# First group's diagonal sums from products by channel on TensorE, and SyncE's loads of later groups in another order

## The reference, cut to what matters

```python
# attention, per batch and head, token by token
kt, vt, rt, wt = k[t], v[t], r[t], w[t]
y[t]  = rt @ (state + outer(u * kt, vt))
state = wt[:, None] * state + outer(kt, vt)
# first block
h = x @ w_in
x = knee(h) @ w_out        # 0 below -1, h above 1, (h + 1)^2 / 4 between
# second block
out = (silu(x @ w_gate) * (x @ w_val)) @ w_out2
```

## Time and profile before

| | us |
|---|---|
| median of 3 runs | 955.78 |
| lowest and highest run | 955.15, 956.08 |
| the profiled execution | 956.56 |
| its span | 954.8 |
| TensorE busy | 934.9 |
| VectorE busy | 553.4 |
| ScalarE busy | 392.3 |
| GpSimd busy | 166.4 |

### The profile page before, as it was taken

One profiled execution on the slowest core, in us unless ns is written; L12 is line 12 of the kernel. 1 busy time (PEld: TensorE's weight loads), 2 busy tenths in 40 slices (PEclk: granted clock), 3 DMA queues, 4 the chain that ended last, 5 costly groups with the idle time before them and its releaser, 6 DMA issues.

```text
span 954.8 us, 20721 instructions
## 1 busy us (share of the span) xinstructions
PE 934.9 (98%) x8344; PEld 918.9 (96%) x8344; DVE 553.4 (58%) x975; ACT 392.3 (41%) x827; POOL 166.4 (17%) x155
## 2 busy tenths in 40 slices
PE   6899999999999999999999999999999999999997
PEld 5889999999999999999999999999999999999997
DVE  8998877777778778764444433333343343434333
ACT  5675545455454555535674322222222222222222
POOL 5993220402104022020444100000000000000000
PEclk9999999999999999999999999999999999999999
DMA  9825453443523435322334010010101001010000
GB/s 306 247 85 181 117 155 117 119 150 116 187 85 116 143 102 161 116 58 88 103 86 119 21 50 1 1 50 1 50 0 49 0 0 49 0 49 0 25 1 27
DMA packets 49715, 79.58 MB, mean 83 GB/s; under 512 B 14784, under 2 KB 35648, under 8 KB 49632
## 3 DMA queue, kind: packets, MB, share of 16 engines
q1 hardware_dynamic: 49632, 78.42, 26.1%
HBM read 60.71 MB, written 17.69 MB: 82 GB/s over the span
## 4 chain that ended last, share of the span: by engine, by line
PE 91%; DVE 5%; issue 2%; ACT 0%; DMA 0%; POOL 0%; DVEq 0%; POOLq 0%
PE bank L1437 50%; PE bank L1465 35%; PE bank L1496 2%; PE bank L1527 2%; PE bank L1522 1%; DVE suf L1130 1%; PE bank L1514 1%; DVE k_r_by_channel L1155 0%; DVE k_r_by_channel L1152 0%; DVE gate L1279 0%; DVE glo L1272 0%; DVE att L1197 0%; DVE diag L1160 0%; DMA w_by_channel<-in_w_channel 0%; DVE att L1203 0%
## 5 line engine op out<-in xcount | busy, mean ns | idle before, releaser
L969 ACT ACTIVATE ghi<-gate 128x384 fp32r<-128x384 f32 x224 | 117.3, 524 | 209.7 <-DVE gate L1291 95.4
L1272 DVE TENSOR_TENSOR glo<-gate,ghi 128x384 fp32r<-128x384 f32 x224 | 136.8, 611 | 83.0 <-ACT ghi L969 81.2
L1289 DVE TENSOR_TENSOR gate<-bank,gate 128x384 f32<-128x384 f32 x96 | 53.5, 558 | 215.0 <-ACT gate L1090 215.0
L1437 PE MATMUL bank<-xhi,w2gv_ahi 128*128 128x384 f32 x480 | 161.3, 336 | 0.0
L1437 PE MATMUL bank<-xlo,w2gv_ahi 128*128 128x384 f32 x480 | 161.3, 336 | 0.0
L1437 PE MATMUL bank<-xhi,w2gv_alo 128*128 128x384 f32 x480 | 161.3, 336 | 0.0
L1090 ACT ACTIVATE gate<-bank 128x384 f32<-128x384 f32 x96 | 47.2, 492 | 227.7 <-PE bank L1437 227.7
L1465 PE MATMUL bank<-ghi,w1ohi 128*128 128x384 f32 x384 | 132.8, 346 | 1.0 <-DVE glo L1272 1.0
L1437 PE MATMUL bank<-xhi,w1ihi 128*128 128x384 f32 x384 | 129.6, 337 | 1.4 <-issue 0.9
L1437 PE MATMUL bank<-xhi,w1ilo 128*128 128x384 f32 x384 | 129.4, 337 | 0.0
L1465 PE MATMUL bank<-glo,w1ohi 128*128 128x384 f32 x384 | 129.4, 337 | 0.0
(11 more groups left out here) (105 smaller groups left out, 1506.6 us busy)
## 6 DMA issues: line engine op xcount, KB each, us to landing
r_k_v_by_token<-in_rkv_token SPq DMA_DIRECT2D x21, 672.0 KB, 5.2
k_r_by_channel<-in_kr_channel SPq DMA_DIRECT2D x18, 512.0 KB, 3.9
w_by_channel<-in_w_channel SPq DMA_DIRECT2D x24, 226.2 KB, 3.6
k_blocks_out<-k_blocks SPq DMA_DIRECT2D x18, 256.0 KB, 2.6
k_moved<-k_blocks_out SPq DMA_DIRECT2D x72, 64.0 KB, 2.0
x_t<-ring SPq DMA_DIRECT2D x8, 576.0 KB, 3.2
x_raw<-x_t SPq DMA_DIRECT2D x8, 576.0 KB, 4.0
ring<-in_w_out SPq DMA_DIRECT2D x21, 192.0 KB, 2.9
```

The costliest lines, as they stand in the source:

```text
L969: e.activation(ghi[j % 2][:, :], gate[j % 2][:, :], ACT.Copy).then_inc(M["hi", ph], 1)
L1272: e.tensor_tensor(glo[j % 2][:, :], gate[j % 2][:, :], ghi[j % 2][:, :].bitcast(F32), ALU.subtract)\
L1289: e.tensor_tensor(q, hid[j % 2][:, 0:T], q, ALU.mult).then_inc(M["t", 2], 1)
L1437: m = e.matmul(out, w_of(a, k), x_of(b_, k), start=start and i == 0, stop=stop and i == total - 1)
```

## The change

For the first group alone the sums are made another way. VectorE multiplies r with k by channel, before either is scaled (`r_times_k`). The product lies in the place of r and k by token, which are no longer loaded for this group. After the four transposes of a KT fill, TensorE makes four more matmuls into the same bank: the product as stationary side, and as moving side two columns of a new input `u_of_head` (112 x 4 x 2 numbers), so that 2 sums per pair of heads come out. ScalarE copies them to `diag` behind its copy of k. GpSimd's two products and VectorE's reduction fall away for this group; chunk 3 goes back to GpSimd.

```diff
+        def r_k_of(w):
+            return tok[0:PR, w, 2 * DM - NPAIR * WIN:2 * DM].rearrange("q (p t) -> q p t", p=NPAIR)
...
-                used = 3 * DM if first(g) else 3 * DM + DM // 2
-                e.dma_start(tok[:, w, 0:used], tok_d[g, w][:, 0:used]).then_inc(ld["tok", w], 16)
+                used = slice(2 * DM, 3 * DM) if first(g) else slice(0, 3 * DM + DM // 2)
+                e.dma_start(tok[:, w, used], tok_d[g, w][:, used]).then_inc(ld["tok", w], 16)
...
             load_kr(0, 1)
+            e.dma_start(pick[:, :, :], pick_d).then_inc(ld["pick"], 16)
             load_tok(0, 0)
-            e.dma_start(uu[:, :], u_d).then_inc(ld["u"], 16)
             load_w(0, 2)
             load_kr(0, 2)
             load_tok(0, 1)
-            load_w1(1)
+            load_w1(2)
             load_tok(0, 2)
-            load_w1(RING - 1)
+            load_w1(RING - 2)
+            e.dma_start(uu[:, :], u_d).then_inc(ld["u"], 16)
...
                 then_load(load_w, 1)
+                then_load(load_kr, 0)
+                then_load(load_tok, 0)
                 move_x(g, 0)
-                then_load(load_kr, 0)
                 move_k(g, 2)
-                then_load(load_tok, 0)
                 then_load(load_w, 2)
+                move_x(g, 1)
+                move_x(g, 2)
                 for w in (1, 2):
-                    move_x(g, w)
                     then_load(load_kr, w)
                     then_load(load_tok, w)
...
-            diag_products(0, 0)
-            diag_products(0, 1)
             diag_values(0, 0)
-            diag_products(0, 2)
+            w1_lo(0)
+            diag_values(0, 1)
+            w1_lo(1)
             decay_second()
-            diag_values(0, 1)
             diag_values(0, 2)
...
                     e.activation(ktk[:, :], src[:, 0:NPAIR * PR], ACT.Copy).then_inc(kt_out, 1)
+                    if first(g):
+                        e.activation(dg[:, w, :], src[:, NPAIR * PR:NPAIR * PR + H], ACT.Copy).then_inc(diag_d, 1)
...
+            more_hi(2)
             drain(0, fill_no(0, "KT", 2), 0)
...
+            def r_times_k(w):
+                e.wait_ge(ld["kr", w], 16)
+                e.tensor_tensor(r_k_of(w), kr[:, w, 1, :, :], kr[:, w, 0, :, :], ALU.mult).then_inc(r_k, 1)
...
             for w in range(2):
                 scan_window(0, w)
+                r_times_k(w)
                 scale_window(0, w)
-            diag_sum(0, 0)
             drain_at(0)
             scan_window(0, 2)
+            r_times_k(2)
             scale_window(0, 2)
...
-            diag_sum(0, 1)
-            diag_sum(0, 2)
             drain_at(2)
...
-            w1_lo(DVE_CHUNK)
             suffix_scan(1, 0)
...
                         m = e.transpose(out[:, p * PR:(p + 1) * PR], kr[:, w, 0, p, :], ident[0:PR, 0:PR])
+                    if first(g):
+                        e.wait_ge(r_k, w + 1)
+                        e.wait_ge(ld["pick"], 16)
+                        for p in range(NPAIR):
+                            c0 = NPAIR * PR + 2 * p
+                            m = e.matmul(out[:, c0:c0 + 2], r_k_of(w)[:, p, :], pick[:, p, :], start=True, stop=True)
```

More of the change, by code:

```diff
@@ L114 @@
 SCAN_SLOTS_FIRST = {11: 0, 13: 1, 14: 2}
-DVE_CHUNK = 3
 HI_FIRST = {0: 13, 1: 13, 2: 15, 3: 18, 4: 21, 5: 24, 6: 27, 7: 30, 8: 32}
@@ L152, in fill_no, with build_program @@
     return fills(g).index((kind, w, n))
-def build_program(nc, w_d, kr_d, tok_d, u_d, cst_d, w1i_d, w1o_d, w2g_d, w2v_d,
+def build_program(nc, w_d, kr_d, tok_d, u_d, pick_d, cst_d, w1i_d, w1o_d, w2g_d, w2v_d,
                   w2o_d, rs_d, ks_d, vs_d, ws_d, us_d, out_d, x2_d, ys_d, kb_d, xb_d):
@@ L233, in build_program @@
         dg, _ = place("diag", [P, NW, H], F32)
+        pick, _ = place("u_of_head", [PR, NPAIR, 2], F32)
         assert at[0] <= flag_at
@@ L271, in sem @@
             return ctx.enter_context(nc.semaphore(name))
-        ld = {n: sem(f"ld_{n}") for n in ("cst", "u")}
+        ld = {n: sem(f"ld_{n}") for n in ("cst", "u", "pick")}
         ld.update({(n, w): sem(f"ld_{n}{w}") for n in ("w", "kr", "tok") for w in range(NW)})
@@ L276, in build_program @@
         raw2 = [sem(f"raw2_{i}") for i in range(RING2)]
-        whi, wlo, wlo_d = sem("whi"), sem("wlo"), sem("wlo_d")
+        whi, wlo = sem("whi"), sem("wlo")
         whi2, wlo2 = sem("whi2"), sem("wlo2")
@@ L284, in build_program @@
         diag_d = sem("diag_d")
+        r_k = sem("r_k")
         fill = sem("fill")
@@ L331, in wait_lo @@
         def wait_lo(wait, c):
-            if c == DVE_CHUNK:
-                wait(wlo_d, 1)
-            else:
-                wait(wlo, c + 1 if c < DVE_CHUNK else c)
+            wait(wlo, c + 1)
         def bank_of(g, f):
@@ L836, in w1_lo @@
             def w1_lo(c):
-                if c == DVE_CHUNK:
-                    return
                 t = w1i if c % 2 == 0 else w1o
@@ L842, in diag_products @@
             def diag_products(g, w):
-                n = (g * NW + w) * OPS_DIAG
+                n = ((g - 1) * NW + w) * OPS_DIAG
                 rk = r_tok(w)
@@ L864, in decay_second @@
                 e.wait_ge(st_out, 2 * w)
-                e.wait_ge(diag_p, NW * OPS_DIAG)
                 for i in range(2):
@@ L872, in decay_second @@
                 e.wait_ge(st_dec, OPS_DECAY * (w + 1))
-            diag_products(0, 0)
-            diag_products(0, 1)
             diag_values(0, 0)
-            diag_products(0, 2)
+            w1_lo(0)
+            diag_values(0, 1)
+            w1_lo(1)
             decay_second()
-            diag_values(0, 1)
             diag_values(0, 2)
             for c in range(2 * J1):
-                w1_lo(c)
+                if c > 1:
+                    w1_lo(c)
                 if c in PRODUCTS_AT:
@@ L1158, in diag_sum @@
             def diag_sum(g, w):
-                e.wait_ge(diag_p, (g * NW + w) * OPS_DIAG + 2)
+                e.wait_ge(diag_p, ((g - 1) * NW + w) * OPS_DIAG + 2)
                 e.tensor_reduce(dg[:, w, :], r_tok(w).rearrange("p (h d) -> p h d", d=D), AX.X, ALU.add)\
@@ L1244, in turn_k @@
                 if n == 0:
-                    e.wait_ge(wlo, 2 * J1 - 1)
-                    e.wait_ge(wlo_d, 1)
+                    e.wait_ge(wlo, 2 * J1)
                 else:
@@ L1304, in _ @@
             e.wait_ge(zero_p, 3)
-            def w1_lo(c):
-                t = w1i if c % 2 == 0 else w1o
-                e.wait_ge(whi, c + 1)
-                e.wait_ge(raw[c % RING], 16 * (c // RING + 1))
-                e.tensor_tensor(t[1][:, c // 2, :], chunk_raw(c), t[0][:, c // 2, :].bitcast(F32),
-                                ALU.subtract).then_inc(wlo_d, 1)
+            def r_times_k(w):
+                e.wait_ge(ld["kr", w], 16)
+                e.tensor_tensor(r_k_of(w), kr[:, w, 1, :, :], kr[:, w, 0, :, :], ALU.mult).then_inc(r_k, 1)
             def drain_at(w):
@@ L1563, in bank_free @@
                     e.wait_ge(kt_out, gg * NW + (w + 1))
+                    if first(gg):
+                        e.wait_ge(diag_d, w + 1)
                 elif kind == "AT":
@@ L1665 @@
     kr_rows = np.stack([by_window(by_channel(inputs[n], 0.0)) for n in ("k", "r")], axis=3)
+    u_of_head = np.zeros((2, 64, NPAIR, 2), np.float32)
+    for i in range(2):
+        u_of_head[i, :D, :, i] = inputs["u"].reshape(NPAIR, 2, D)[:, i].T
     arrays = {
@@ L1670 @@
         "u_row": np.ascontiguousarray(np.broadcast_to(inputs["u"].reshape(1, DM), (P, DM))),
+        "u_of_head": np.ascontiguousarray(u_of_head.reshape(P, NPAIR, 2)[:PR]),
         "constants": cst,
```

## The result

| | before | changed |
|---|---|---|
| median | 954.84 | 957.36 |
| lowest and highest, 20 runs each | 953.38, 957.65 | 954.12, 960.37 |
| the profiled execution | 956.56 | 954.12 |

The ratio is 1.0023 (1.0015 to 1.0031): 2.2 us slower, 1.4 to 3.0. The prediction had said 954.4, a change of -1.4, and at most 957.2. The forecast stood on the median of three runs, 955.78; twenty runs of the kernel before give 954.84, so its profiled execution (956.56) is 1.7 above the median.

What follows compares the result with a forecast made beforehand. TensorE, busy 934.9 of 954.8 us, was taken as the bound. The first stage's +0.7 and SyncE's order at -2.1 summed to -1.4, from 955.78 to 954.4 us, range 952.9 to 957.2.

Steps and rivals of the forecast that it cites:

- I take the weight half of the transpose, 0.109: First group's KT fills: each two-column matmul record costs 0.109 us, giving +0.9 at KT1 and +0.5 at KT2.
- KT0 gets 0.9 too, covered by VectorE: First KT fill: its new matmuls also cost 0.9 us, but hidden behind VectorE's work.
- VectorE up to KT1, +1.3: First stage: `r_times_k` in two windows and a collision with GpSimd's product with v start KT1 1.3 us later.
- the 0.4 set against it: Same VectorE term up to KT1, 0.4 us if VectorE and GpSimd only shared instead of excluding each other.
- The waits that vanish, -1.4: TensorE from KT1 to XT0: waits for VectorE, ScalarE and GpSimd vanish as TensorE comes later, -1.4 us.
- XT0 at 27.85: End of the first stage: XT0 starts at 27.85 us, 1.3 later than before.
- The rival with TensorE slow for longer: First stage: the clock rises only after Y2, KT2's transposes still take 1.01, total 958.4 us; chance 0.12.
- Into the first slots, -0.6: Behind the last drain: VectorE's chunk 3 (0.56 us) is gone ahead of the knee TensorE waited for, -0.6 us.
- SyncE's order, -2.1: Later groups: the new load order removes TensorE's holes at 124 and 252 us, -1.3 and -0.8, bounds 0 and -2.1.
- its first rival (0.27): Later groups: the holes stay or come up elsewhere, only the start counts, 956.5 us; chance 0.27.
- a hole of about 1 us in another group: Later groups: a TensorE hole of this size elsewhere would show the prediction wrong.
- Behind the loads: Holes at 124 and 252 us: TensorE was read as out of instructions because its fetches stood behind loads.

Runs made afterwards that it cites:

- n_none: Changed kernel without the twelve two-column matmuls, ScalarE copying eight columns of k instead of the sums: 953.27 us, ratio 0.9983 to the kernel before.
- n_fp32r: Changed kernel with the two-column matmuls on numbers rounded to fp32r, one record each instead of two: 952.60 us, ratio 0.9981 to the kernel before.
- n_again: The changed kernel run again, unchanged, for another profile: 957.14 us, ratio 1.0019 to the kernel before.
- b_sp: The kernel before with only the new order of loads in later groups: 954.51 us, ratio 0.9997 to the kernel before.
- n_again2: The changed kernel run unchanged once more, with the last experiments: 957.00 us, ratio 1.0025 to the kernel before.
- n_early: Changed kernel with eleven matmuls of zeros on TensorE ahead of the first fill: 953.19 us, ratio 0.9982 to the kernel before.
- b_early: The kernel before with eleven matmuls of zeros on TensorE ahead of the first fill: 956.13 us, ratio 1.0008 to the kernel before.
- n_early_pick: Changed kernel with eleven early matmuls of zeros and `u_of_head` loaded third instead of sixth: 952.87 us, ratio 0.9976 to the kernel before.

## Why the prediction was wrong, point by point

Two steps of the prediction failed: the price of a two-column record, and the holes that SyncE's order was to remove. From -1.4 to the +2.2 of the ratio are 3.6 us: 2.1 for the holes, 1.2 for the first stage (its end 2.5 later, not 1.3), 0.2 at the knee.

- **"I take the weight half of the transpose, 0.109" failed.** Eight records of two columns took 1.73 to 1.84 us at the slow level and 0.96 at the fast, 0.22 and 0.12 each: the whole price of a transpose record, the upper end that the text had named and not taken. That is 0.8 more than the term at KT1 and 0.4 more at KT2. The Trainium skill (TensorE: Matmul & The Clock Gate, "LDWEIGHTS") gives a weight load's time by its columns alone, about 107 ns for 128; the records at the fast level agree with that, those at the slow level take double.
- **"KT0 gets 0.9 too, covered by VectorE" failed with it.** KT0 has 1.8 and a wait of 0.3 to 0.4 for `u_of_head`, and both are on the path: TensorE was ready for KT1 at 13.70, VectorE at 12.12. With 0.9 at KT0, TensorE would have been ready at 12.8 and still the later one. Together the prices are some 2.1 us too little: 0.9 at KT0, 0.8 at KT1, 0.4 at KT2. TensorE now sets the end. In n_none and n_fp32r, where the records are fewer, the first `tile_in` is 2.7 us earlier; their medians are 3.9 and 4.5 lower (3.4 and 3.6 by the ratios), and the late holes have a part in that.
- **VectorE up to KT1, +1.3:** the sum itself gives 12.95 - 11.71 = 1.2, and the 0.4 set against it is the case without any loss; if the 0.75 stood again, the term would be 1.2 as well. The mechanism holds, the place doesn't. The sums of KT0 came at 11.7, not 10.8, for the same reason as above, so GpSimd met L1159 and nobody waited for it. `r_times_k` cost its 0.59. KT1 was 2.1 late in n_again, for TensorE. In n_none, where ScalarE's copies come early, the collision is there as described.
- **The waits that vanish, -1.4:** they went, as said, and were larger: XT0 of n_again is 2.5 late, by 2.1 at KT1, 1.7 and 0.9 for the records behind it, less 2.2. In the fast profile a wait for ScalarE came instead (0.60 before ST1, its `diag`), not in n_again.
- **XT0 at 27.85:** 29.02 in n_again and 25.82 in the profile after, the fastest execution of twenty, which is luck. The rival with TensorE slow for longer was given 0.12 and tied to KT2 at 1.01. KT2 took 0.55 in all three profiles of the changed kernel as it is, so the rival as put is out. What it had right is that the fills of the changed kernel hang on the clock: the rise came at 22.1 to 23.2 against 20.8 and 21.7. Before, 0.9 of a later rise moved nothing (b_sp), as VectorE set the end; in the changed kernel 1.1 us of it moved the first `tile_in` by 0.6 (n_again2, n_again) and 8.6 us by 3.2. That is a part of the spread of 954 to 960, how large a part three traces don't tell.
- **Into the first slots, -0.6:** -0.4, the wait for the knee from 0.59 to 0.17.
- **SyncE's order, -2.1:** failed, and by its size it is the larger of the two. The two holes went, and as many came elsewhere. The text had this as its first rival (0.27), with the right reason, that the records added at the start move each fetch, and had named "a hole of about 1 us in another group" as a sign of being wrong: it stands at 241 us. For the sum it took the other. The reading "TensorE out of instructions" is borne out by the step of 256 records. "Behind the loads" is open: the order is worth 0 to 0.8 us, and the hole at 251 left the profile of b_sp without a gain in its median.
- **The sum** with what n_again shows: 2.1 + 1.7 + 0.9 - 2.2 = +2.5 at XT0 and at the first `tile_in`, -0.4 at the knee, 0 for the holes: +2.1, for -1.4. Measured were +2.5 between the medians and +2.2 by the ratio. That the holes count 0 rests on the one trace of the kernel before. The two traced executions are only 0.7 apart (956.56 and 957.23): the matmuls from 126 to 162 us take 0.7 us longer in that of the kernel before, without a wait, and for this and the rest of the difference no cause was found.

## What to carry to other kernels

A small fp32 matmul costs two full records: with 128 stationary columns, two moving columns were as dear here as 128, so a sum of eight numbers a token cost as much on TensorE as eight transposes; fp32r halves it where the rounding can be borne. (No run has fewer stationary columns.) Work that is moved to TensorE before its clock has risen is paid at double price, and where TensorE becomes the bound of such a stage the kernel's time begins to depend on when the clock rises: profile more than one execution before reading it. Before a hole without a releaser is credited to an edit, count TensorE's records up to it: here it stood at the same remainder by 256 in every trace, and any edit that adds instructions in front moves it.

## What the runs showed of the hardware

- The clock fell back about short stands: to 0.50 at 11.0 us in n_early after a wait of 1.69 us, at 11.9 in b_early after one of 1.39, at 12.3 in n_early_pick during one of 2.02, and then TensorE worked for 7 to 10 us at the slow level before it rose again (21.3, 22.1, 19.2).
- The same instructions at nearly the same times led to a rise at 14.6 us in one execution and at 22.1 and 23.2 in two others.
- 28 late stops of TensorE, of 0.19 to 1.34 us in 20 traces, all stand where its count of matmul and weight-load records leaves 193 or 194 by 256.
- Twelve transposes ahead of the rise aren't needed for it (14.6 came before any of them), but without them it came at 29.9, the latest of all. The Trainium skill (TensorE: Matmul & The Clock Gate, "Part 4: PE-mode transpose") says that transposes don't engage the gate; the late rise without them speaks against it, in one profile.
- Sixteen TensorE records of no use at the start made the changed kernel 1.8 us faster by the medians, 0.9 by the ratios, and two of its three late stops were gone.
